# Network 1's output by tokens, in pairs of blocks, its result turned through a scratch in memory

## The reference, cut to what matters

```python
# x: (2, 4096, 192), weight: (8, 7); 8192 tokens in all
w = softmax(weight)                                  # 7 taps for each of 8 heads of 24 channels
attn = causal_convolution_over_tokens(x, w)          # out[s, c] = sum_k w[head(c), k] * x_pad[s + k, c]
g = attn @ w_gate                                    # 192 -> 1536
y = (g * sigmoid(g) * (attn @ w_val)) @ w_out1       # 1536 -> 192
h = y @ w_in2                                        # 192 -> 2048
out = where(h > 0, h, exp(min(h, 0)) - 1) @ w_out2   # 2048 -> 192
```

## Time and profile before

| | |
|---|---|
| time, median of 3 runs | 1204.67 us (1204.64 to 1207.97) |
| profiled execution, its own time | 1206.76 us |
| its span, first to last instruction | 1205.0 us |
| granted TensorE clock | 1.000 (of 2.4 GHz) |
| TensorE busy | 1199.5 us, 11798 matmuls |
| VectorE, ScalarE, GpSimd busy | 775.5, 664.2, 717.9 us |
| DMA | 43.37 MB, 103955 packets, of which 75888 under 512 B |

### The profile page before, as it was taken

The page is one execution under the profiler, slowest core; times in us unless marked ns, Lnnn a source line. Parts: engine busy times, 40 slices in busy tenths (PEclk is TensorE's granted clock), DMA queues, the critical chain, the costliest instruction groups (busy, mean ns, idle before and its releaser), DMA issues.

```text
span 1205.0 us, 31390 instructions
## 1 busy us (share of the span) xinstructions
PE 1199.5 (100%) x11798; PEld 1032.4 (86%) x11798; DVE 775.5 (64%) x1178; ACT 664.2 (55%) x1114; POOL 717.9 (60%) x528
## 2 busy tenths in 40 slices
PE   9999999999999999999999999999999999999999
PEld 7988888888888888889888898888988889888898
DVE  6787575675656756567665666656666476675665
ACT  6456555465554645546455464655546556465565
POOL 6787656574654746547465474654746557465565
PEclk9999999999999999999999999999999999999999
DMA  7412012120111211012110121100212002120110
GB/s 179 109 51 44 12 27 41 32 44 11 32 31 30 44 30 23 21 30 44 30 27 17 30 44 30 35 17 22 44 30 41 11 22 44 30 44 9 30 34 15
DMA packets 103955, 43.37 MB, mean 36 GB/s; under 512 B 75888, under 2 KB 93936, under 8 KB 103920
## 3 DMA queue, kind: packets, MB, share of 16 engines
q1 hardware_dynamic: 103104, 42.29, 15.7%
q10 hardware_dynamic: 816, 0.59, 0.2%
HBM read 16.12 MB, written 6.29 MB: 19 GB/s over the span
## 4 chain that ended last, share of the span: by engine, by line
PE 97%; POOL 1%; DVE 1%; issue 1%; ACT 0%; ACTq 0%; DVEq 0%
PE up L860 55%; PE down L860 42%; POOL hid_lo L441 1%; DVE mixed L830 0%; DVE act L771 0%; PE down L1063 0%; POOL up_w_lo L326 0%; DVE hidden L787 0%; ACT L617 0%; ACT hid_hi L608 0%; POOL y_main L445 0%; POOL halves L445 0%; DVE mixed L827 0%; DVE taps_head L813 0%; ACT act L593 0%
## 5 line engine op out<-in xcount | busy, mean ns | idle before, releaser
L441 POOL TENSOR_TENSOR hid_lo<-hidden,hid_hi 128x512 fp32r<-128x512 f32 x447 | 623.7, 1405 | 473.2 <-ACT hid_hi L574 304.8
L860 PE MATMUL down<-out_w,hid_hi 64*128 64x384 f32 x2040 | 300.4, 355 | 0.0
L734 DVE TENSOR_TENSOR hidden<-act,up 128x512 f32<-128x512 f32 x191 | 130.8, 685 | 249.1 <-ACT act L557 249.1
L860 PE MATMUL down<-out_w,hid_lo 64*128 64x192 f32 x2040 | 260.8, 251 | 0.3 <-POOL hid_lo L441 0.3
L771 DVE TENSOR_SCALAR act<-up 128x512 f32<-128x512 f32 x256 | 164.8, 685 | 112.0 <-PE up L860 112.0
L860 PE MATMUL up<-in_b_hi,up_w_hi 64*128 64x512 f32 x1128 | 224.1, 393 | 0.0
L860 PE MATMUL up<-in_b_hi,up_w_lo 64*128 64x512 f32 x1128 | 223.7, 393 | 0.0
L860 PE MATMUL up<-in_b_lo,up_w_hi 64*128 64x512 f32 x1128 | 223.6, 393 | 0.0
L574 ACT ACTIVATE hid_hi<-hidden 128x512 fp32r<-128x512 f32 x192 | 121.5, 633 | 177.9 <-DVE hidden L734 160.5
L608 ACT ACTIVATE hid_hi<-hidden 128x512 fp32r<-128x512 f32 x256 | 156.9, 628 | 96.5 <-DVE hidden L787 79.4
L593 ACT ACTIVATE act<-act 128x512 f32<-128x512 f32 x256 | 156.1, 631 | 94.8 <-DVE act L771 94.8
(11 more groups left out here) (96 smaller groups left out, 1085.9 us busy)
## 6 DMA issues: line engine op xcount, KB each, us to landing
x_raw<-x_dram SPq DMA_DIRECT2D x136, 64.0 KB, 2.2
out_dram<-stage SPq DMA_DIRECT2D x15, 384.0 KB, 2.7
in_b_hi<-in_b_hi SPq DMA_DIRECT2D x32, 128.0 KB, 2.3
in_b_lo<-in_b_lo SPq DMA_DIRECT2D x32, 128.0 KB, 2.3
swapped<-halves SPq DMA_DIRECT2D x32, 128.0 KB, 2.3
in_a_hi<-in_a_hi SPq DMA_DIRECT2D x30, 128.0 KB, 2.3
in_a_lo<-in_a_lo SPq DMA_DIRECT2D x30, 128.0 KB, 2.3
stage<-w_out_dram SPq DMA_DIRECT2D x7, 384.0 KB, 3.9
```

The lines of the kernel that those rows point to most:

```text
L441: return pool.tensor_tensor(hid_lo[:, slot, :], hidden[:, s, :], hid_hi[:, slot, :].bitcast(F32), ALU.subtract)
L734: v.tensor_tensor(hidden[:, f % 2, :], act[:, f % 2, :], val_bank(f, n)[:, :], ALU.mult)\
L860: return nc.tensor.matmul(dst, lhsT, rhs, start=start, stop=stop, skip_group_check=True)
```

## The change

Network 1's output is computed as network 2's is. `out1_w` has the layout of `out2_w`: 192 high columns and 192 low. `down1` is replaced by `down1_pair`, which takes two blocks f0 and f0 + 1 over four turns of banks as `down2_pair` does, with the hidden block stationary. A pair follows the `project` of each even f from 4 on, the pair (8, 9) that of f = 11, and the pair (10, 11) the first `project` of the next `elu_phase`. ScalarE copies the low columns of the four banks to `y_tok` (`copy_y`), VectorE adds the high columns to it (`add_y`, which waits for each copy), and GpSimd's three additions are gone. SP stores `y_tok` by tokens to a scratch `y_rows` in memory (`store_y`), waits for that, and loads it as it loads x, in 8 DMAs (`load_y`), in place of `swap_halves`. VectorE turns both parts by transposes (`turn_y`) at f = 2, 3 of the next mix phase (f = 6, 7 for chunk 0, j = 4, 5 of `elu_phase(15)` for the last). For the last chunk `input2_hi` and `input2_lo` come one j later. `down2_pair(n - 1, 0)` now waits for `y_done`, VectorE's additions.

```diff
         def out1_piece(q):
-            out_piece(wo1_rows, out1_w, q, [(D, P, TAIL), (D + TAIL, 0, P)], "pool")
+            out_piece(wo1_rows, out1_w, q, [(D, 0, D)], "pool")
...
-            def swap_halves(n):
-                sp.wait_ge(halves_done, n + 1)
-                if not is_int(n, 0):
-                    sp.wait_ge(y_tail_done, n)
-                for to, of in ((0, TAIL), (TAIL, 0)):
-                    sp.dma_start(swapped[to:to + TAIL, :], halves[of:of + TAIL, :]).then_inc(swap_done, 16)
+            def store_y(n):
+                sp.wait_ge(y_done, BLOCKS * (n + 1))
+                sp.dma_start(y_tokens, y_tok[:, :, :]).then_inc(y_stored, 16)
+
+            def load_y(n):
+                sp.wait_ge(y_stored, 16 * (n + 1))
+                for part in range(2):
+                    for q in range(BANDS):
+                        channel = P + q * B % TAIL if part else q * B
+                        sp.dma_start(y_raw[q * B:(q + 1) * B, part, :].rearrange("i (n d) -> i n d", d=B),
+                                     y_blocks[:, :, channel:channel + B]).then_inc(y_loaded, 16)
...
             with sp.Fori(1, CHUNKS - 1) as n:
-                swap_halves(n)
-
+                store_y(n)
+                load_y(n)
                 load_x(n + 3, (n + 3) & (CHUNKS - 1))
...
             def copy_y(n):
                 a.wait_ge(down1_done, N1 * (n + 1))
                 if not is_int(n, 0):
-                    a.wait_ge(y_tail_done, n)
-                nc.scalar.activation(halves[:, :], TAIL_A[:, :], ACT.Copy).then_inc(y_a, 1)
-                if not is_int(n, 0):
-                    a.wait_ge(in2_lo, 2 * n)
-                nc.scalar.activation(y_main[:, :], MAIN_A[:, :], ACT.Copy).then_inc(y_a, 1)
+                    a.wait_ge(y_stored, 16 * n)
+                for b in range(BLOCKS):
+                    nc.scalar.activation(y_tok[:, b, :], BY_TOKENS[b][:, D:2 * D], ACT.Copy).then_inc(y_a, 1)
...
-            def copy_y(n):
-                v.wait_ge(down1_done, N1 * (n + 1))
+            def add_y(n):
+                for b in range(BLOCKS):
+                    v.wait_ge(y_a, BLOCKS * n + b + 1)
+                    v.tensor_tensor(y_tok[:, b, :], y_tok[:, b, :], BY_TOKENS[b][:, 0:D], ALU.add)\
+                        .then_inc(y_done, 1)
+
+            def turn_y(n, part):
+                v.wait_ge(y_loaded, 16 * 2 * BANDS * (n + 1))
                 if not is_int(n, 0):
-                    v.wait_ge(y_main_done, n)
-                v.tensor_copy(halves_b[:, :], TAIL_B[:, :]).then_inc(y_b, 1)
-                v.tensor_copy(y_main_b[:, :], MAIN_B[:, :]).then_inc(y_b, 1)
+                    v.wait_ge(in2_lo, 2 * (n - 1) + 1 + part)
+                v.transpose((y_main, y_tail)[part][:, :], y_raw[:, part, :]).then_inc(y_turned, 1)
...
+                    at = 6 if is_int(n, 1) else 2
+                    if f in (at, at + 1) and not is_int(n, 0):
+                        turn_y(n - 1, f - at)
...
-                    if j in (5, 6) and is_int(n, CHUNKS - 1):
-                        input2_lo(n, j - 5)
+                    if j in (4, 5) and is_int(n, CHUNKS - 1):
+                        turn_y(n, j - 4)
+                    if j in (6, 7) and is_int(n, CHUNKS - 1):
+                        input2_lo(n, j - 6)
...
+            def by_tokens(w, k, data, b, b_low, start, stop):
+
+                columns = slice(0, 2 * D) if data is hid_hi else slice(0, D)
+                w, slot = w[:, k, columns], k % RING
+                mm(BY_TOKENS[b][:, columns], data[TOP, slot, b * P:b * P + P], w[TOP], start, stop)
+                return mm(BY_TOKENS[b_low][:, columns], data[LOW, slot, b_low * P:b_low * P + P], w[LOW], start, stop)
...
+            def down1_pair(n, f0):
+                turns = 2 * (N1 // 2 * n + f0 // 2)
+                if f0 == 0 and is_int(n, 0):
+                    pe.wait_ge(mul_done, LAG)
+                elif f0 == 0 and is_int(n, 1):
+                    pe.wait_ge(y_done, BLOCKS)
+                elif f0 == 0:
                     pe.wait_ge(result_done, summed(n - 1))
...
+                for turn, (b, b_low) in banks_of_pair(f0):
+                    if turn >= 2:
+                        pe.wait_ge(y_turn, turns + turn - 1)
+                    for f in (f0, f0 + 1):
+                        pe.wait_ge(hi1_done, N1 * n + f + 1)
+                        by_tokens(out1_w, f, hid_hi, b, b_low, f == 0 and b < 2, False)
+                        pe.wait_ge(lo1_done, N1 * n + f + 1)
+                        end = by_tokens(out1_w, f, hid_lo, b, b_low, False, f == N1 - 1 and b < 2)
+                    if turn < 2:
+                        end.then_inc(y_turn, 1)
+                end.then_inc(down1_done, 2)
...
-                    if f >= LAG:
-                        if chunk0 and f - LAG in OUT1_AT:
-                            wait_weights(pe, OUT1_AT[f - LAG])
-                        if chunk0 and f == LAG:
-                            pe.wait_ge(mul_done, LAG)
-                        down1(n, f - LAG)
+                        down1_pair(0, N1 - 2)
+                    if f >= RING and f % 2 == 0:
+                        if chunk0 and f - RING in OUT1_AT:
+                            wait_weights(pe, OUT1_AT[f - RING])
+                        down1_pair(n, f - RING)
                     if f == N1 - 1:
-                        down1(n, N1 - LAG)
+                        if chunk0 and N1 - RING in OUT1_AT:
+                            wait_weights(pe, OUT1_AT[N1 - RING])
+                        down1_pair(n, N1 - RING)
```

More of the change, by code:

```diff
@@ L29, with mix_ffn_ffn @@
 P = 128
-def mix_ffn_ffn(nc, x, weight, w_gate, w_val, w_out1, w_in2, w_out2, out):
+def mix_ffn_ffn(nc, x, weight, w_gate, w_val, w_out1, w_in2, w_out2, out, y_rows):
     BATCH, SEQ, D = x.shape
@@ L119, in mix_ffn_ffn @@
         hid_lo = sb("hid_lo", [P, RING, T], F32R)
-        y_main, y_main_b = sb("y_main", [P, T]), sb("y_main_b", [P, T])
-        halves, halves_b = sb("halves", [P, T]), sb("halves_b", [P, T])
-        swapped = sb("swapped", [P, T])
+        y_tok = sb("y_tok", [P, BLOCKS, D])
+        y_raw = sb("y_raw", [P, 2, T])
+        y_main = sb("y_main", [P, T])
         y_tail = sb("y_tail", [P, T])
@@ L202, in mix_ffn_ffn @@
         hi2_done = sem("hi2_done")
-        y_main_done = sem("y_main_done")
         y_a = sem("y_a")
-        y_b = sem("y_b")
+        y_done = sem("y_done")
+        y_turned = sem("y_turned")
+        y_turn = sem("y_turn")
         z_a = sem("z_a")
@@ L480, in elu_phase @@
                     lo_of(k % 2, k % RING).then_inc(lo2_done, 1)
-                    if k == 3 and not last:
-                        sum_y_tail(n)
-                    if k == 5 and not last:
-                        sum_y_main(n)
-                    if k == 9 and not last:
-                        fold_y_tail(n)
                     if k % 2:
@@ L789, in elu_phase @@
                     if j == 0:
-                        add_z(n - 2) if last else copy_y(n)
+                        add_z(n - 2) if last else add_y(n)
                     extra(j)
@@ L934, in down2_pair @@
                 elif k0 == 0:
-                    pe.wait_ge(y_a, 2 * (m + 2))
-                    pe.wait_ge(y_b, 2 * (m + 2))
-                order = ((0, 2), (1, 3), (2, 0), (3, 1))
-                for turn, (b, b_low) in enumerate(order if k0 // 2 % 2 == 0 else order[::-1]):
+                    pe.wait_ge(y_done, BLOCKS * (m + 2))
+                for turn, (b, b_low) in banks_of_pair(k0):
                     if turn >= 2:
                         pe.wait_ge(z_turn, turns + turn - 1)
-                    for k in two:
+                    for k in (k0, k0 + 1):
                         pe.wait_ge(hi2_done, N2 * m + k + 1)
-                        by_tokens(k, hid_hi, b, b_low, first=k == 0)
+                        by_tokens(out2_w, k, hid_hi, b, b_low, k == 0 and b < 2, False)
                         pe.wait_ge(lo2_done, N2 * m + k + 1)
-                        end = by_tokens(k, hid_lo, b, b_low, last=k == N2 - 1)
+                        end = by_tokens(out2_w, k, hid_lo, b, b_low, False, k == N2 - 1 and b < 2)
                     if turn < 2:
@@ L1039, in elu_phase @@
                     elif j == 0:
-                        down1(n, N1 - 2)
-                        down1(n, N1 - 1)
+                        down1_pair(n, N1 - 2)
                     if j >= 2:
```

95 lines of the change are left out of this document (24 added, 71 removed).

## The result

The changed kernel takes 1235.94 us (median of 4 runs, 1232.9 to 1238.26) against 1204.66: ratio 1.0252, 95% interval 1.0223 to 1.028. The forecast was 1202.7, in a range of 1199.5 to 1208. The profiled execution took 1232.9 us around a span of 1231.2; the one of before took 1206.76 around 1205.0.

The account below looks back on a forecast made before the run. TensorE's stream was taken to bound the kernel. Steady chunks -2.7 us, first chunk +0.7 and end +0.1 summed to -1.9, say -2: 1202.7 us against the median of 1204.67, in a range of 1199.5 to 1208.

Parts of the forecast that it names:

- rival 4: Start and end: VectorE slips, second network's weights or longer program's fetch hold TensorE; +2 to +6, 1204.7 to 1208.7; chance 0.15.
- the sum of the forecast: Whole kernel: -2.7 + 0.7 + 0.1 = -1.9, say -2 us, giving 1202.7 against the median of 1204.67.
- What bounds the kernel: Whole span: TensorE bounds, busy 1199.5 of 1205.0 us, chain 97% on it; only its stream's length or waits matter.
- The steady stream: TensorE, steady chunks: 74.14 us becomes 73.96, 0.18 less each; -2.7 us over fifteen of sixteen chunks.
- rival 2: Mix phase: a pair costs by columns, 2.10 us, saving 0.23 on each of 96 pairs: 1182 us; chance 0.03.
- Rival 1: All 16 chunks gain 0.18 and nothing is lost, pairs perhaps cheaper still: 1198.9 to 1201.8 us; chance 0.12.
- The first chunk: Chunk 0: the last pair waits for late `hid_lo` and ends at 56.2, before 55.48; +0.7 us, bounds 0 and 2.
- The end: Last chunk: `input2_hi` and `input2_lo` one j later might delay the last P group by 0 to 0.5 us; 0.1 taken.
- The y path and the added wait: Y back 9.9 us after its last addition; `y_done` at 617.6 with 1.3 us of room: no cost.
- rival 3: Steady chunks: y evacuation outlasts its window, 10.5 us in 15 chunks: 1213, or 1206 if a third are hit; chance 0.10.

Follow-up runs that it names:

- slot 72: Changed kernel with TensorE's loop head at place 72 of a block of 256 instructions, ending five instructions before the seventh block's end: 1205.97 us, ratio 1.0.
- 88: Changed kernel with TensorE's loop head at place 88 of a block of 256 instructions, ending eleven inside the eighth block: 1237.36 us, ratio 1.0261.
- experiment 5: Changed kernel with the loop's branch back announced by a hint: 1205.92 us unplaced, 1206.23 with the head at place 200, 1205.4 at place 88.
- slot 200: Changed kernel with TensorE's loop head at place 200 of a block of 256 instructions, touching eight blocks: 1263.42 us, ratio 1.0467.
- after_slot0: Changed kernel with TensorE's loop head at the start of a block of 256 instructions, touching seven blocks: 1205.93 us, ratio 0.999.
- the padded old stream: Kernel before with 160 instructions of always-true waits added per TensorE lap: 1225.5 us with the head at place 0 of a block, 1261.67 at place 200.

## Why the prediction was wrong

**The step that failed** is the term that rival 4 held at arm's length: "the fetch of a longer program" was priced, with the weights and VectorE's slip, at +2 to +6, and the text says that 1152 matmuls more are "priced by nothing in the trace"; the sum of the forecast holds nothing for it. What the runs showed in its place: in a straight line the longer program is fetched at no cost that can be told, but the lap as it came to lie is fetched anew at 4 of its 12 branches back, and each time TensorE stops and its clock falls, 26.8 us in all. The profile had the row from which to ask. The page of before has 24 packets on its instruction queue for a program that runs 11798 matmuls and as many loads, so its loop was held and not fetched anew: a body that fits is free, and the question is how near the edge it is. The working counted matmuls for their time and never as instructions of a lap (736 to 808, 1549 to 1715). The rule on taken branches of the Trainium skill (Runtime: NRT & Kernel Launch, Instruction fetch mechanics, quoted above) was not weighed either; taken as it stands it asks for a fetch at each branch of both kernels, and the kernel before shows none. By the 2048 instructions that the same section gives, the new lap alone would still have fitted. What decides is the place of the head (slot 72 against 88), and, as argued in experiment 5, a block fetched ahead. A fair rival would have been: the loop no longer fits, up to twelve laps, each with a wait for a block and a granted clock that falls behind it. By the runs of the changed stream this is 27 us (unplaced) to 59 us (slot 200) with a bad head and nothing with a good one, depending on an address that the diff doesn't show.

**What bounds the kernel**: right. In the versions without stops TensorE is busy for 1198 us of 1204.2 and the chain lies 97% on it.

**The steady stream**: right in kind, a third too large. The order that the prediction writes out for the mix phase (five P ahead of the first D2) is that of chunk 0; in a steady chunk two D2 of network 2 stand behind f = 0 and 1, and its counts, 14 D2 and 6 other P, are those of the steady chunk. The pair in the mix phase takes 2.28 us, D2's price, so rival 2 (cost by columns, 1182) is refuted. Of after_slot0:

```profile
584.29 0.37 PE L841 MATMUL down<-out_w,hid_hi 64*128 64x384 f32 x2
...
586.57 0.45 PE L841 MATMUL up<-in_b_hi,up_w_hi 64*128 64x512 f32 x2
...
590.77 0.37 PE L841 MATMUL down<-out_w,hid_hi 64*128 64x384 f32 x2
```

The three P in a row of each steady mix phase (f = 2 to 4) stand in the chain as one piece of 54 matmuls, once a chunk (start, us, what):

```profile
208.15 6.31 PE up L841 x54
...
1096.23 6.31 PE up L841 x54
```

Twelve chunks in 888.08 us are 74.007 each, against 73.96 forecast and 74.13 before: -0.12 and not -0.18 a chunk, -1.9 over fifteen and not -2.7. The pieces were read to 0.01 us, and a difference of 0.06 over 34 pieces is what such rounding leaves; the difference was built from small rests of large numbers. Rival 1 (0.18 gained in all 16 chunks and nothing lost) fails by this and by the start.

**The first chunk**: +0.7 forecast (0 to 2), about +2.2 measured. The mechanism was right and named: the last pair waits for `hid_lo`, 0.55 us, and chunk 0's stream ends at 56.84 where 56.2 was forecast and 55.48 was before. The pair began at 54.01 and not at 53.5, and GpSimd's last `hid_lo` of the chunk ended at 54.88, 0.7 later than the 54.17 taken over from before. Missed was what comes behind it, 0.85 us in chunk 1: the y copies on ScalarE now stand behind a late pair and in front of the gate of f = 2, at the one place where a weight piece stands there too. The text had written "Nothing" for ScalarE, from a steady chunk.

**The end**: right, in that no wait of TensorE stands in it. **The y path and the added wait**: as forecast. From after_slot0, the rows that answer to the earlier trace rows:

```profile
616.17 0.97 ACT L512 ACTIVATE y_tok<-down 128x192 f32<-128x192 f32 x4
616.52 1.15 DVE L684 TENSOR_TENSOR y_tok<-y_tok,down 128x192 f32<-128x192 f32 x4 [1.00 <-ACT y_tok L512]
```

The additions end at 617.67, forecast 617.6, and take the 1.15 us of `add_z`; no matmul of a steady chunk waits for them, so rival 3 (1206 to 1213) is refuted. The trip through memory, in the DMA issues of the changed kernel (KB, us to landing), cost no more than assumed:

```profile
y_raw<-y_rows SPq DMA_DIRECT2D x128, 64.0 KB, 2.3
y_rows<-y_tok SPq DMA_DIRECT2D x16, 384.0 KB, 2.5
```

**The sum without the stops**: 1205.9, in the range and 3 us above the forecast: 0.8 us of it is the steady term, 1.5 the start. The remaining part is the base: the median of three runs that it was set against, 1204.67, lay at the lowest of several levels (executions of the kernel before run from 1204.4 to 1207.9), and in all later measurements the kernel before stood at 1205.9 to 1206.9. In spans, 1205.0 to 1204.2, the steady stream and the start come to -1.9 + 2.2 = +0.3, where -0.8 was measured. The rest is a stall that only the profiled execution of the kernel before has, in `elu_phase(1)`; it includes the wait for `hid_lo` of the earlier trace rows:

```profile
119.19 0.50 PE L860 MATMUL up<-in_a_hi,up_w_hi 64*128 64x512 f32 x2 [0.40 <-DVE hidden L787]
...
122.32 0.36 PE L860 MATMUL down<-out_w,hid_lo 64*128 64x192 f32 x2 [0.31 <-POOL hid_lo L441]
```

With its loop written out the same kernel has neither wait, and from there on it is 1.3 us earlier (span 1203.7). So with the stops out of the way the change is worth about nothing: the steady gain of 1.9 is used up by the start.

## What to carry to other kernels

When a change adds instructions to a rolled loop, count the instructions of one lap for each engine and the blocks of 256 that they touch from the loop's head, and read the instruction queue of the profile: packets that move while the laps run mean that the loop is fetched anew. An idle engine with "issue" as its releaser, at the place of a branch back, is this cost, and a hint at the branch or a placed head removed it here entirely, without touching the work. An expected gain of a quarter of a per cent is smaller than what such a border, or two engines meeting once at the start, takes.

## What the runs showed of the hardware

- TensorE kept a loop that touches seven blocks of 256 instructions (slots 0 and 72), or eight with the branch hinted (slot 200), through 12 branches with no packet moved. An eighth block without the hint cost nine packets in each lap that was fetched anew and a stop of 2.0 to 4.8 us.
- The granted clock fell to 0.50 at each stop of the changed kernel and of slots 88 and 200 (2.7 to 4.8 us idle), which cost some 2 us more a stop. With the padded old stream (2.0 to 2.3 us idle) it fell behind only 4 of 12 stops.
- The stop was longest when the branch stood just inside the eighth block (3.9 to 4.4 us at slot 88, and 4.3 to 4.8 in the changed kernel, which seems to lie there), though it then came only 4 or 5 times of 12; further inside it came each time and took 2.7 to 3.4 us (slot 200), or 2.0 to 2.3 with the padded old stream.
- Waits that always hold aren't free on a busy TensorE, and their price depends on what runs ahead of them: 8 such instructions ahead of a P cost 0.11 to 0.24 us where the P followed short matmuls (384 and 192 columns), and 0.02 or less where it followed 512-column ones; 18.7 us in the span.
- Fetching 103 packets in a straight line cost nothing that can be told (1205.9 against 1205.93 with 27).
